# Where VectorE splits the attention output and turns the key blocks: a fused linear-attention and two-FFN kernel on one Trainium2 core

## The reference

```python
# attention: B, H, S, D = 2, 8, 768, 48
for t in range(S):
    cur = einsum('bhd,bhe->bhde', u * k[t], v[t])
    y[t] = einsum('bhd,bhde->bhe', r[t], state + cur)
    state = w[t][..., None] * state + einsum('bhd,bhe->bhde', k[t], v[t])
x = y reshaped to (1536 tokens, 384)
# first FFN, ELU: w_in (384, 2048), w_out (2048, 384)
h = x @ w_in
x = where(h > 0, h, exp(min(h, 0)) - 1) @ w_out
# four dense experts, ReLU: w1 (384, 1024), w2 (1024, 384) each
p = probs / (probs.sum(-1) + 1e-9)
out = sum over e of p[:, e] * (max(x @ w1[e], 0) @ w2[e])
```

## Time and profile before

| what | value |
|---|---|
| median of 3 runs | 647.96 us (647.87 to 648.05) |
| the profiled execution, its own time | 647.89 us |
| its span (first to last instruction) | 646.1 us |
| TensorE busy | 639.0 us (99%) |
| VectorE busy | 418.1 us (65%) |
| GpSimd busy | 295.6 us (46%) |
| ScalarE busy | 238.2 us (37%) |

### The profile page before, as it was taken

One profiled execution on the slowest core, in us unless ns is written; L12 is line 12 of the kernel. 1 busy time (PEld: TensorE's weight loads), 2 busy tenths in 40 slices (PEclk: granted clock), 3 DMA queues, 4 the chain that ended last, 5 costly groups with the idle time before them and its releaser, 6 DMA issues.

```text
span 646.1 us, 13797 instructions
## 1 busy us (share of the span) xinstructions
PE 639.0 (99%) x5044; PEld 592.0 (92%) x5044; DVE 418.1 (65%) x786; ACT 238.2 (37%) x561; POOL 295.6 (46%) x370
## 2 busy tenths in 40 slices
PE   8999999999999999999999999999999999999998
PEld 5998999877788888999999999999999999999997
DVE  7888988965357666655565656565656565656564
ACT  4776555645445554222222222222222222222221
POOL 5897424420499999996019900019900019000000
PEclk9999999999999999999999999999999999999999
DMA  8953454300000133100012100012100011001011
GB/s 323 403 196 131 137 167 175 121 18 1 1 2 1 56 102 99 40 1 1 1 50 98 50 1 0 1 49 98 50 1 0 0 50 50 0 1 49 0 50 50
DMA packets 19043, 42.34 MB, mean 66 GB/s; under 512 B 2608, under 2 KB 8752, under 8 KB 18992
## 3 DMA queue, kind: packets, MB, share of 16 engines
q1 hardware_dynamic: 18704, 41.23, 18.5%
q10 hardware_dynamic: 288, 0.39, 0.2%
HBM read 37.16 MB, written 4.46 MB: 64 GB/s over the span
## 4 chain that ended last, share of the span: by engine, by line
PE 89%; POOL 5%; DVE 3%; issue 1%; DMA 0%; ACT 0%; POOLq 0%; DVEq 0%
PE bank L1351 29%; PE bank L1352 28%; PE bank L1353 28%; POOL w_lo L549 4%; PE bank L1197 1%; PE bank L1266 1%; DVE fr L870 1%; PE bank L1278 1%; DMA rkw<-rkw_dram 0%; DVE att L928 0%; DVE fr L889 0%; PE bank L1222 0%; POOL tok L530 0%; DVE bank L1001 0%; PE bank L1286 0%
## 5 line engine op out<-in xcount | busy, mean ns | idle before, releaser
L1351 PE MATMUL bank<-x_lo,w_hi 128*128 128x256 f32 (+2 forms) x416 | 138.2, 332 | 0.6 <-DVE w_lo L971 0.3
L1352 PE MATMUL bank<-x_hi,w_lo 128*128 128x256 f32 (+2 forms) x416 | 135.2, 325 | 0.0
L1353 PE MATMUL bank<-x_hi,w_hi 128*128 128x256 f32 (+2 forms) x416 | 135.2, 325 | 0.0
L1352 PE MATMUL bank<-w_hi,g_lo 128*128 128x384 f32 x384 | 129.6, 337 | 0.0
L1353 PE MATMUL bank<-w_hi,g_hi 128*128 128x384 f32 x384 | 129.3, 337 | 0.0
L1351 PE MATMUL bank<-w_lo,g_hi 128*128 128x384 f32 x384 | 129.0, 336 | 0.0
L833 ACT ACTIVATE g_hi<-bank 128x512 fp32r<-128x512 f32 x96 | 57.5, 599 | 144.3 <-DVE bank L1057 122.4
L1351 PEld LDWEIGHTS bank<-x_lo,w_hi 128*128 128x128 f32 x416 | 78.2, 188 | 10.6 <-issue 2.6
L1353 PEld LDWEIGHTS bank<-x_hi,w_hi 128*128 128x128 f32 x416 | 78.3, 188 | 7.4
L1352 PEld LDWEIGHTS bank<-x_hi,w_lo 128*128 128x128 f32 x416 | 78.3, 188 | 7.1
L1050 DVE TENSOR_TENSOR u_sum<-p_copy,bank 128x256 f32<-128x256 f32 x56 | 23.6, 421 | 92.1 <-ACT p_copy L757 91.4
(11 more groups left out here) (133 smaller groups left out, 1259.6 us busy)
## 6 DMA issues: line engine op xcount, KB each, us to landing
raw<-w_dram SPq DMA_DIRECT2D x48, 384.0 KB, 3.7
rkw<-rkw_dram SPq DMA_DIRECT2D x10, 772.5 KB, 4.5
tok<-tok_dram SPq DMA_DIRECT2D x10, 576.0 KB, 6.2
k_blocks_dram<-k_blocks SPq DMA_DIRECT2D x8, 256.0 KB, 4.1
kt_sb<-k_blocks_dram SPq DMA_DIRECT2D x32, 64.0 KB, 2.0
out_dram<-acc SPq DMA_DIRECT2D x10, 192.0 KB, 1.9
rkw<-rkw_dram SPq DMA_DIRECT2D x2, 512.0 KB, 4.5
rkw<-rkw_dram SPq DMA_DIRECT2D x2, 260.5 KB, 3.2
```

What stands on the lines that cost most here:

```text
L1351: pe.matmul(out, wh, ml, start=start, stop=False, skip_group_check=shared)
L1352: pe.matmul(out, wl, mh, start=False, stop=False, skip_group_check=shared)
L1353: return pe.matmul(out, wh, mh, start=False, stop=stop, skip_group_check=shared)
```

## The change

Only VectorE's order changes; every engine issues the same instructions as before.

- `lo_x(c)`, for chunks that don't end a tile (c = 2, 4, 5, 6, 8, 9, 10, 11), moves within its step from ahead of `elu(n)` to behind `lo_g(n)`, the half low parts of `LO_AFTER` and the late turns. For c = 3 and 7 it stays.
- The blocks of the fourth chunk (c = 3) are turned in step 11, behind `lo_g(11)`, and no longer at the end of step 10. Late turns now stand ahead of `bonus`.
- Half low part (14, 0) moves from behind `lo_g(12)` to between `elu(12)` and `lo_g(12)`, and (14, 1) from behind `lo_g(14)` to behind `lo_g(13)`.
- In step 17 `lo_x2` of the first tile moves from behind both halves of `mask_scores(4)` to between them.

```diff
--- before.py
+++ after.py
@@ -92,16 +92,17 @@
 SCALE_R = {c: step - 1 for c, step in SCORES.items() if c > FIRST}
 SCALE_R_FIRST = 6
 
-TURNS = {c: step for c, step in SCALE_K.items() if c < NC - B}
-LATE_TURNS = {c: SCORES[c] - 1 for c in TILE_STARTS if FIRST < c < NC - B}
+LATE_TURNS = {c: SCORES[c] - 1 for c in (FIRST + 1, *TILE_STARTS) if FIRST < c < NC - B}
+TURNS = {c: step for c, step in SCALE_K.items() if c < NC - B and c not in LATE_TURNS}
 
 
 HALF_TILES = 2
 PAST_TURN = (0, 1, 4) * 5 + (0, 1, 0, 1) + (2, 0, 1) * 4 + (2,)
 NUPDATE = NC - B
 
-LO_BETWEEN = {1: ((5, 0),), 2: ((5, 1),), 3: ((3, 1),), 4: ((8, 0),), 5: ((8, 1),), 6: ((10, 0),), 7: ((10, 1),)}
-LO_AFTER = {11: ((13, 0),), 12: ((14, 0),), 14: ((14, 1),)}
+LO_BETWEEN = {1: ((5, 0),), 2: ((5, 1),), 3: ((3, 1),), 4: ((8, 0),), 5: ((8, 1),), 6: ((10, 0),), 7: ((10, 1),),
+              12: ((14, 0),)}
+LO_AFTER = {11: ((13, 0),), 13: ((14, 1),)}
 LO_VECTOR = [(2, 0), (2, 1)] + [half for step in range(J1) for half in LO_BETWEEN.get(step, ()) + LO_AFTER.get(step, ())]
 LO_LAST = [(15, 0), (13, 1), (15, 1)]
 LO_POOL = [(n, half) for n in range(J1) for half in range(2) if (n, half) not in LO_VECTOR + LO_LAST] + LO_LAST
@@ -1061,18 +1062,17 @@
                 dve.tensor_tensor(in_halves(bank[1][:, :]), in_halves(bank[1][:, :]), twice(u3), ALU.add).then_inc(s_c, 1)
 
             for n in range(SINGLE):
+                past = n // J1 - 1
                 for c in due(n, 1):
                     mask_scores(c, 0, BESIDE)
+                    if n == J1 + LAG - 1:
+                        lo_x2(past, blocks_of(past)[0])
                     mask_scores(c, 1, BESIDE)
                 for c in due(n, 3):
-                    if c < NUPDATE and c + 1 not in TILE_STARTS:
+                    if c + 1 in TILE_STARTS:
+                        lo_x(c, BESIDE["y"])
+                    if c < NUPDATE:
                         add_update(c, BESIDE)
-                    lo_x(c, BESIDE["y"])
-                    if c < NUPDATE and c + 1 in TILE_STARTS:
-                        add_update(c, BESIDE)
-                past = n // J1 - 1
-                if n == J1 + LAG - 1:
-                    lo_x2(past, blocks_of(past)[0])
                 elu(n)
                 if n == 0:
                     add_update(0, BANKS0)
@@ -1098,10 +1098,13 @@
                     add_update(1, BANKS1)
                 for half in LO_AFTER.get(n, ()):
                     lo_w(*half)
+                for c in due(n, 0, LATE_TURNS):
+                    turn_blocks(c)
+                for c in due(n, 3):
+                    if c + 1 not in TILE_STARTS:
+                        lo_x(c, BESIDE["y"])
                 for c in due(n, -1):
                     bonus(c)
-                for c in due(n, 0, LATE_TURNS):
-                    turn_blocks(c)
                 for c in due(n, 0, PRODUCTS):
                     products(c)
                 for part in range(2):
```

## The result

The changed kernel takes **653.01 us** (median of 6 runs, 652.31 to 653.19), the kernel before, beside it on the same chip, 647.83 (647.74 to 648.05): 1.0076 times as long, interval 1.0065 to 1.0087. It is slower, as forecast, but by 5.2 us instead of 2.7, and outside the range of 650.0 to 652.7. The profiled execution took 653.0 us with a span of 651.2.

What follows compares the result with a forecast made beforehand. TensorE, busy 639.0 of 646.1 us, bounds the kernel, so only its waits count. -1.3 + 4.0 = +2.7 us on the profiled 647.89 gives 650.6, with the median 0.07 above: 650.7 us; 8 in 10 range 650.0 to 652.7.

Steps and rivals of the forecast that it cites:

- both terms of its sum: A gain of 1.3 us up to step 19 and a loss of 4.0 us at early_up(0).
- The early gain of 1.3 us: Waits shortened or closed in steps 12 to 18 gain 1.3 us up to step 19; bounds 0.3 and 2.0.
- (a): TensorE's wait at scores(3) for scale_r(3), 0.93 us behind the matmul before; forecast gone, at most 0.82 us.
- (d): TensorE's wait for lo_x2 at the third block of down1(16): loses 0.53 us, forecast to close, with 0.1 us of restart.
- (b): TensorE's wait at up(14), after lo_w(14, 0): up(14) forecast at 51.53, a gain of 0.86 us together with (a).
- `lo_x` of the other chunks: Later by up to a step; only the next chunk's outputs wait on them, at least a step away.
- Chunk 3's blocks: Turned later, they land at 55.3, 0.1 us ahead of update(3); DMAs 0.5 us slower would cost 0.4 us.
- the wait of 4.0 us: At early_up(0): lo_x(11) starts 4.99 us later, so TensorE waits 3.92 us plus 0.1 restart; bounds 3.6 and 4.3.
- The clock falls in the pause: Rival, chance 0.20: clock drops to 1.2 GHz at the early_up(0) pause, costing up to 2.3 us more, 653.0 at most.
- the opening fillers: Nearest row for the clock fall's length: 8 opening matmuls of 384 columns, read as 4.6 us at the lower level.
- the early gain not being there: Rival, chance 0.11: late chunk 3 blocks or slower GpSimd bonus products leave 0.3 us of gain: 651.7 us.
- the late `lo_x(11)` is covered: Rival, chance 0.04: lo_x(11) late by less than 1.12 us, so only the gain stands: 646.7 us, faster.

Runs made afterwards that it cites:

- e1: The changed kernel with only lo_x(11) put back ahead of elu(44): 646.62 us, ratio 0.9982 to the kernel before.
- e5: e1 with lo_x2 of step 17 back behind both masks: 647.24 us.
- e6: e1 with half low parts (14, 0) and (14, 1) back at their old places: 647.18 us.
- e7: e1 with the turn of chunk 3 back at the end of step 10: 646.66 us, ratio 0.9984.
- e10: e1 with the turn of chunk 3 and every lo_x at their old places: 647.43 us.
- e3: The changed kernel with 17 unused filler matmuls of 512 columns ahead of early_up(0): 650.65 us, ratio 1.0042.
- e2: The kernel before with only lo_x(11) moved late, behind lo_g(44): 653.92 us, ratio 1.009.
- e4: The changed kernel with lo_x(11) directly behind elu(44), ahead of lo_g(44): 650.73 us, ratio 1.0039.

## Why the prediction was wrong

The direction and both terms of its sum held. The time missed by 2.3 us because the sum had nothing in it for the clock: a fall of the clock was a rival that the prediction named, priced and put at 0.20.

**The early gain of 1.3 us: right in size, only in part by its path.** e1 measures 647.86 - 646.62 = 1.24 us. Wait (a) is gone, `scores(3)` starting at 47.82, and `up(14)` starts 0.77 us earlier (51.62; forecast 51.53). It waits there for 0.37 us where before it waited 0.28; the prediction had said less. `up(16)` came 1.03 us earlier (58.15; forecast 58.33), but `scores(4)`, which the prediction didn't look at, gave part of it back: it starts 0.63 us earlier (60.99 against 61.62), as `scale_r(4)` holds it. VectorE's `scale_r(4)` in after and before:

```profile
59.85 1.08 DVE L913 TENSOR_TENSOR rkw<-rkw,fr 128x512 f32<-128x512 f32 x1
```

```profile
60.88 0.68 DVE L912 TENSOR_TENSOR rkw<-rkw,fr 128x512 f32<-128x512 f32 x1
```

It starts 1.03 us earlier and takes 0.40 longer. The prediction moved instructions and kept their lengths; here an instruction that came earlier met one of GpSimd's: the products L531 run from 58.78 to 60.39, beside the moved `scale_r(4)`, while before they had ended at 60.23. The moved `lo_w(14, 0)` starts 1.05 us earlier and takes 0.88 us instead of 0.59, beside GpSimd's L539 (50.42 to 51.96). That the overlap is the cause is read from the rows; no run changes it alone. Then (d) brought its 0.53, and `up(19)` started at 68.62 (forecast near 68.4), 1.12 us earlier than before. The other 0.2 us of after come between `scores(6)` (85.05, 1.13 earlier) and `scores(7)` (97.00, 1.31 earlier); in e1 they are missing, as `update(6)` starts 0.37 us behind the matmul ahead of it, and in after 0.22.

Of the edits, `lo_x2` between the masks is worth 0.6 (e5; forecast 0.63) and the two half low parts 0.6 (e6; forecast 0.86, of which `scores(4)` passes on 0.6). The turn is worth nothing (e7), which the prediction's own reading says: GpSimd's products stand behind (a) and (b) together.

**`lo_x` of the other chunks, costed at nothing: wrong.** The list of waits of before has none at `scores(5)` to `scores(7)`, so I priced their `lo_x` only by who waits for it, and not by what it had held up. With TensorE 1.1 us ahead `scale_r` is what it would wait for next, and the new place of `lo_x` avoids that: 0.8 us (e10 against e7), of which the starts of `scores(5)`, `scores(6)` and `scores(7)` show 0.33, 0.20 and 0.21. It is a part of the 1.3, not an addition; the shares of the single edits overlap and don't add up to it.

**Chunk 3's blocks, costed at nothing with 0.1 us of margin: they are on the edge.** In after `update(3)` has no wait. In e1's profiled execution it starts at 55.81, 0.3 us later, and in e3's it waits a whole microsecond; TensorE and SyncE in e3:

```profile
56.72 0.55 PE L1225 MATMUL bank<-tok,kt_sb 128*32 128x48 f32 x32 [0.99 <-DMA kt_sb<-k_blocks_dram]
```

```profile
49.49 0.33 SPq L458 DMA_DIRECT2D k_blocks_dram<-k_blocks  x1
53.33 1.75 SPq L463 DMA_DIRECT2D kt_sb<-k_blocks_dram  x4
```

The write is 1.2 us later than in after (48.28), as the turn is: it starts at 47.55 in after and at 48.76 in e3 (48.69 in e1), where `scale_r(3)` took 1.09 us and not 0.69. And it is 3.84 us from write to reads where after has 2.91 (48.28 to 51.19). Later waits took most of it up in that execution, and e3's median isn't that run.

**`lo_x(11)` and the wait of 4.0 us: right.** The shift is 4.98 us (forecast 4.99), the wait 3.9 by start times (forecast 3.92), `early_up(0)` starts at 188.63 (forecast 190.00 - 1.3 = 188.7), and e3 against e1 gives 4.0 us for the pause.

**The failed step: "The clock falls in the pause (chance 0.20)", and the range that cut its upper part off.** In the sum the clock stood at nothing, and e3 shows 2.4 us for it. The rival's mechanism was right, its price of at most 2.3 us nearly so, and its time of 653.0 is what was measured. Its chance was wrong. I took the missing case in the trace of before (no pause of 4 us in mid-kernel) as if it spoke against the fall, when it spoke for nothing, and the only rows at hand, the opening fillers, pointed to 4.6 us at the lower level. They do so by their lengths alone: from 2.43 to 5.63 they start 0.64 us apart and take 0.85 us, and the last takes 0.49, while the granted clock reads 1.00 there (0 to 6.5 us, before and after). The runs put in its place: with a pause of 3.9 us the mean clock was at 0.995 or 0.997 in all 6 runs of after and all 4 of e2, and with 2.6 us in four of the five of e4 (0.997). The Trainium skill, page "TensorE: Matmul & The Clock Gate", section "HAM oscillation — how this bites in real kernels", has this case (matmuls, a wait, the return at the half clock); the trace agrees at 3.9 us, and in e4 the clock fell after 2.6 us too, in four runs of five.

The range has a slip beside it: its lower end, 650.0, takes the gain at its bound of 2.0 and the wait at 4.0. With the wait's own lower bound of 3.6 it would be 649.6. Nothing measured hangs on that.

What was left as a rival, the early gain not being there, fell with e1; that the late `lo_x(11)` is covered fell with the list of waits.

## What to carry to other kernels

A chain that costs nothing stands in no list of waits: before its head is moved, subtract its end from the start of what needs it (here 1.12 us for a move of 5). On a kernel whose TensorE is busy for 99%, price a pause of some microseconds in mid-kernel as its length and the half clock behind it (here 3.9 + 2.4 and 2.6 + 1.7), and if the pause can't be avoided, fill it with matmuls that nobody reads. When an engine gets ahead, look at what it would wait for next, not only at the waits in the old list. And don't count on a moved instruction to keep its length (`scale_r(4)`: 0.68 us before, 1.08 after).

## What the runs showed of the hardware

**The clock can fall after the pause.** In e4 it fell 1.1 us after matmuls had resumed, in after and e2 about 1.4 and 1.0 us before they did. The time at half was 6.8 us in the profiled executions of after and e2 and 3.4 in e4's. After's runs lie at 652.3 and 652.4 (two) and at 653.0 to 653.2 (four), e2's at 653.3 and 653.5 and at 654.4 and 654.5. The mean clock was 0.997 in the faster and 0.995 in the slower ones, but for one of after's slower runs: how long the fall lasts seems to vary between runs of one kernel. Against e3's 650.65 us the fall cost about 1.7 us in after's faster runs and 2.4 in the slower. The moments of the fall and the return are from one execution of each kernel.

**Two engines that start together.** At 27.9 us before and after have still run the same program, and yet VectorE's scan there takes 1.13 us in one and 0.70 in the other. VectorE and GpSimd before:

```profile
27.89 1.13 DVE L889 TENSOR_TENSOR_SCAN fr<-rkw,inv_end 128x260 f32<-128x260 f32 x1
```

```profile
27.12 1.34 POOL L549 TENSOR_TENSOR w_lo<-raw,w_hi 128x192 fp32r<-128x192 f32 x2
```

and after:

```profile
27.78 0.70 DVE L890 TENSOR_TENSOR_SCAN fr<-rkw,inv_end 128x260 f32<-128x260 f32 x1
```

```profile
27.02 1.85 POOL L550 TENSOR_TENSOR w_lo<-raw,w_hi 128x192 fp32r<-128x192 f32 x2
```

GpSimd's second low part starts within 0.02 us of the scan in both (at 27.87 and at 27.78). Where GpSimd's two low parts take 1.34 us, the scan has 0.43 more, and where the scan is short, they take 0.51 more: one of the two is held while the other works. The Trainium skill, page "SBUF — State Buffer", section "🔬 SBUF: two separate sides", says that VectorE with two inputs in SBUF and GpSimd lock a shared port pair for a whole instruction, whoever starts first; these rows agree in that one of them is held, but for less (0.43 and 0.51 us) than the other's whole instruction (0.60 and 0.70). Which of them wins changed between executions of programs that are the same up to there (e5 and e10 read like after, the other eight like before), and shifts VectorE by 0.4 us in the steps behind. It is a likely cause of the spread of e1's runs (646.5 to 647.1), but that was not tried.
